# Chunk 0 of a decaying linear attention: outputs summed in banks laid out as x's tiles, state by GpSimd, turned q in a tile of its own

## The chip, the cores and the metric

One core of one Trainium2 chip. The metric is the device time of one execution in microseconds (us), median of 3 runs. Engines are named as in the profile: PE is TensorE, DVE VectorE, ACT ScalarE, POOL GpSimd, SP SyncE.

## The reference

Three stages in fp32, each feeding the next.

```python
# q, k, v, alpha: (4 batches, 8 heads, 768 steps, 48)
for t in range(S):
    state = alpha[:, :, t, :, None] * state + einsum('bhd,bhe->bhde', k[:, :, t], v[:, :, t])
    y[:, :, t] = einsum('bhd,bhde->bhe', q[:, :, t], state)
x = y.transpose(0, 2, 1, 3).reshape(3072, 384)
h = x @ w_in;  x = (relu(h) ** 2) @ w_out        # w_in 384 x 2048, w_out 2048 x 384
h = x @ w2_in; out = (h * sigmoid(h)) @ w2_out   # the same shapes
```

## The kernel before

**Units, chunks, pairs.** The 768 steps are cut into 6 chunks of 128. A chunk of all 4 batches is one unit of 512 tokens, and x of a unit is 384 x 512: KD = 3 tiles of 128 rows, numbered 0 to 2. The 8 heads are taken as 4 pairs, the last heads first, so pair number n = 4 * chunk + place runs from 0 to 23 (PAIRS = 4; places 0 to 3 hold heads 6 and 7, 4 and 5, 2 and 3, 0 and 1).

**Attention of one pair.** Stage A turns alpha so that features lie on partitions (rows 0 to 47 for the first head, 64 to 111 for the second), scans it to the running decay (L1031), and takes the reciprocal in two halves (L1044, into `rcp`). K and Q turn k and q and multiply them by the reciprocal and the decay (L1060 and L1068). For pairs 0 to 3 the turning is done by PE (L582) into banks; from pair 4 on by DVE (L1017), and turned q goes into `rcp`. S is the score product (L615, two banks, one per head); ACT copies it (L835) and POOL masks it for pairs 0 to 2, DVE masks it (L1074) from pair 3 on. T turns scaled k back (L625, copied by L840). I is the sum of k and v for the state (L636), Y the output: scores times v (L661), and from pair 4 on the state times q before it (L657). ACT copies Y's bank to `y_sb` (L846).

**ACT's guards.** ACT squares and sums the decay (`bound_decay`, L822) and the reciprocal (`bound_reciprocal`, L827) to know whether the numbers were in range; both are checks for a fallback at the end. The turned q overwrites `rcp`, so `kq_stage` waits for `bound_reciprocal` first (L1063, `2 * (n + 1)` from pair 4 on).

**How y becomes x.** SP moves `y_sb` to the rows of `x_raw` by small transfers (`repack`, L377): eight for pairs 0 to 2 of chunk 0. Pair 3 of chunk 0 alone is summed straight in the place that it has in x's tile 0 (L649): v lies in a tile with zeros between the two heads, so one stationary operand of 96 columns puts head 0 in rows 0 to 47 and head 1 in rows 48 to 95, and zeros add nothing. x is then split into a high part (ACT) and the rest (DVE, L1117), since each product of the two feed-forward stages is done as three (high high, high low, low high).

**Feed-forward.** A unit has 16 steps. Step F does `first_product` of block F (L675, 9 products of 128x128x512, in the order of tiles 2, 1, 0), ACT takes relu and square (L885, L887, L890, L893), DVE the low part (`low_g`, L1125), and two steps later `second_product` (L689) adds into three banks. The second feed-forward follows after all six units, and is not touched.

**Weights of the first feed-forward** come in five groups (`WGROUPS`, `load_first`): group 0 issued by ACT, groups 1 to 4 by POOL (L333, L335). A chunk is one block of one matrix: ACT copies it to the high part (L860), POOL subtracts (`low_first`, L509). Chunk 2F is wanted by step F, chunk 2F + 1 by step F + 2.

**Order around the change.** What each engine does before step 0 is written out by hand: PE by `AHEAD`, then a piece of the first products, then Y and T of pair 3; ACT, DVE and POOL by their own lists. From step 0 on `stage_step` gives the step in which a stage of pair n is issued. Pairs 4 to 7 have A at 1, 4, 7, 10, K and Q at 3, 6, 9, 12, S at 4, 7, 10, 13 and I and Y one step after S; pair 8 has A at 12, K and Q at 13, S at 15, I and Y at 16. On PE a stage stands between the first and the second product of its step (S of pair 4 stands behind the second). DVE's `s_stage`, `i_stage`, `state_stage` and `kq_stage` stand ahead of `low_g` of the step, its A behind it. An engine runs its list strictly in order.

Of the kernel before, what the change touches and what calls it, by code (L numbers as in the profile page):

```python
# [38 lines left out]
AHEAD = [("A", 0), ("A", 1), ("K", 0), ("Q", 0), ("S", 0), ("T", 0), ("K", 1), ("A", 2), ("Q", 1), ("I", 0), ("Y", 0),  # L39
# [6 lines left out]
EDGE = 2 * HD  # L46
# [30 lines left out]
def early_chunks(f):  # L77

    if f < 2:
        return range(6 + 3 * f, 9 + 3 * f)  # L80
    return range(8 + 2 * f, min(10 + 2 * f, NCHUNK))
# [7 lines left out]
def y_count(n):  # L89

    return n if n < PAIRS else n - 1
# [25 lines left out]
def moved(units, pair):  # L117

    per_pair = [len(repack_pieces(p)) for p in range(PAIRS)] + [0] * 2
    unmoved = per_pair[PAIRS - 1] if pair % 2 and not is_first(units) else 0  # L120
    whole = sum(per_pair[pair % 2::2])
    if is_first(units):
        return 16 * sum(per_pair[pair % 2:pair:2])
    return 16 * (whole * (units - 1) + whole + sum(per_pair[pair % 2:pair:2]) - unmoved)
# [20 lines left out]
def build(nc, q, k, v, alpha, w1_in, w1_out, w2_in, w2_out, out):  # L145
    z_dram = nc.dram_tensor("z_scratch", (UNITS, DM, UT), F32, kind="Internal").ap()
    ctx = ExitStack()
    with ctx:
# [15 lines left out]
        w_raw = [sb(f"w_raw{i}", [P, DM], F32) for i in range(RING)]  # L164

        x_raw = sb("x_raw", [P, KD, UT], F32)
        x_hi = [sb(f"x_hi{i}", [P, KD, UT], F32R) for i in range(2)]
# [56 lines left out]
        v_wide = z_sb[:, 0:BATCH * 3 * HD].rearrange("p (b x d) -> p b x d", b=BATCH, x=3)  # L224

        v_third = z_sb[:, BATCH * 3 * HD:BATCH * 5 * HD].rearrange("p (b x d) -> p b x d", b=BATCH, x=2)

        def v_tile(n):
            return {PAIRS - 2: v_third, PAIRS - 1: v_wide[:, :, 0::2, :]}.get(n, v_sb[n % 2][:])

        def a_bank(n):
            return z_ps[n % 2]

        def i_bank(n):
            return [z_ps[2], h_ps[1], z_ps[0], z_ps[1]][n] if n < PAIRS else job_ps[1]
# [3 lines left out]
        v_in = [sem(f"v_in{i}") for i in range(2)]  # L239
        a_made, k_made, q_made, kt_made = sem("a_made"), sem("k_made"), sem("q_made"), sem("kt_made")  # L240
# [16 lines left out]
        edge_hi, edge_lo = sem("edge_hi"), sem("edge_lo")  # L257
# [68 lines left out]
        CONSTS, PADS, GEN_CONSTS = 13, 7, 11  # L326
# [21 lines left out]
        def _(sp):  # L348
# [21 lines left out]
            def load_v(n):  # L370
                if n >= PAIRS:
                    wait(sp, y_made, n - 1)
                load_pair("v", n // PAIRS, n % PAIRS, v_tile(n), v_in[n % 2])
# [99 lines left out]
        def _(pool):  # L473
            def load_chunk(n, src, total):
                wait(pool, w_hi_made, total - RING + 1)
                wait(pool, w_lo_made, total - RING + 1)
                dst = w_raw[n % RING][:]
# [11 lines left out]
            nc.gpsimd.memset(v_wide[:, :, 1, :], 0.0).then_inc(consts, 1)  # L489
            pool.wait_ge(consts, 11)  # L490
# [20 lines left out]

            ends(0)
# [11 lines left out]
            ends(3)  # L524
            mask(2)
            load_first(pool, 2)
# [3 lines left out]
            pool.wait_ge(edge_hi, 1)  # L530
            nc.gpsimd.tensor_tensor(x_lo[0][EDGE:, 0, :], x_raw[EDGE:, 0, :], x_hi[0][EDGE:, 0, :].bitcast(F32),
                                    ALU.subtract).then_inc(edge_lo, 1)
            pool.wait_ge(edge_lo, 1)
            low_first(4)
            low_first(5)

            pool.wait_ge(x_hi_made, KD)
            for i in range(3, len(WGROUPS)):
                load_first(pool, i)
            low_first(6)  # L540
            low_first(7)

            for n in range(PAIRS, 2 * PAIRS):
                at = 8 + 6 * (n - PAIRS)
                pool.wait_ge(end_made, n + 1)
                for c in range(at, at + 3):
                    low_first(c)
                pool.wait_ge(rcp_made, 2 * (n + 1))
                low_first(at + 3)
                pool.wait_ge(q_scaled, n + 1)  # L550
                for c in range(at + 4, at + 6):
                    low_first(c)
            for n in range(NCHUNK, 2 * NCHUNK):
# [24 lines left out]
        def _(pe):  # L578
# [8 lines left out]

            def a_stage(n):
                loaded("a", n)

                wait(pe, scanned, BATCH * (n - 1))
# [13 lines left out]
            def s_stage(n):  # L605

                wait(pe, k_scaled, n + 1)
                wait(pe, q_scaled, n + 1)
                wait(pe, y_copied, y_count(n))
# [11 lines left out]
            def t_stage(n):  # L621
                if has_state(n):
                    wait(pe, kt_copied, n)
                    for b in range(BATCH):
# [3 lines left out]
            def i_stage(n):  # L628
                wait(pe, kt_copied, n + 1)
                wait(pe, v_in[n % 2], 32 * (n // 2 + 1))  # L630
                if n < PAIRS:
                    wait(pe, scanned, BATCH * (n + 1))
                else:
                    wait(pe, masked, 2 * n + 1)
                for b in range(BATCH):
                    last = nc.tensor.matmul(i_bank(n)[0:ROWS, b * 2 * HD:(b + 1) * 2 * HD], kp_t[:, b, :],  # L636
                                            v_tile(n)[:, b], start=True, stop=True)
                last.then_inc(i_made, 1)

            def y_stage(n):  # L640

                wait(pe, v_in[n % 2], 32 * (n // 2 + 1))
                wait(pe, masked, 2 * (n + 1))
                ps, p = job_ps[2], n % PAIRS
                if n == PAIRS - 1:

                    for b in range(BATCH):
                        for h in (0, 1):
                            last = nc.tensor.matmul(ps[0:EDGE, tile(b)], v_wide[:, b, h:h + 2, :].rearrange("p x d -> p (x d)"),  # L649
                                                    score[h][:, b, :], start=(b == 0 and h == 0), stop=(h == 1),  # L650
                                                    skip_group_check=True)
                    last.then_inc(y_made, 1)
                    return
                if n >= PAIRS:
                    wait(pe, state_made, 2 * (n - PAIRS + 1))
                    for b in range(BATCH):
                        nc.tensor.matmul(ps[0:ROWS, tile(b)], state[:, p, b, :], qp[n % 2][:, tile(b)],  # L657
                                         start=(b == 0), stop=False, skip_group_check=True)
                for b in range(BATCH):
                    for h in (0, 1):  # L660
                        last = nc.tensor.matmul(ps[head_rows(h), tile(b)], v_tile(n)[:, b, h, :], score[h][:, b, :],  # L661
                                                start=(n < PAIRS and b == 0), stop=True, skip_group_check=True)
# [48 lines left out]
            pe.wait_ge(consts, CONSTS)  # L711
            for kind, n in AHEAD:
                stage(kind, n)
# [559 lines left out]
```

## Time and profile before

| | us |
|---|---|
| runs | 934.92, 932.99, 932.90: median 932.99 |
| the profiled execution, its own time | 936.0 |
| its span in the profile | 934.4 |
| PE busy | 902.1 (97%), weight loads 749.9 |
| DVE busy | 440.7 (47%) |
| ACT busy | 403.0 (43%) |
| POOL busy | 78.3 (8%) |

The profile is of one execution; engines run side by side, so busy times don't add up. What bounds the time is the engine whose idle time is smallest, and each idle stretch of it has to be read by what ended it.

### The profile page before, as it was taken

What the parts mean: (1) busy time and instruction counts of PE and PEld (TensorE: products, weight loads), DVE (VectorE), ACT (ScalarE), POOL (GpSimd) and SP (SyncE); (2) the same over time, 40 slices, a digit from 0 to 9 for tenths busy, and PEclk for the clock granted to TensorE, in tenths of its full rate; (3) what the DMA queues carried; (4) which work ended last, traced back from release to release, by engine and by line L of the source; (5) the groups of instructions that cost most, each with busy time, mean ns of one, the idle gap of its engine ahead of it and who ended that gap; (6) DMA issues with size and microseconds to landing.
All of it is one profiled execution on the core that took longest, in us unless ns stands there. A gap on an engine that the chain in (4) does not pass through costs nothing.

```text
span 934.4 us, 12573 instructions
## 1 busy us (share of the span) xinstructions
PE 902.1 (97%) x4722; PEld 749.9 (80%) x4722; DVE 440.7 (47%) x666; ACT 403.0 (43%) x750; POOL 78.3 (8%) x115
## 2 busy tenths in 40 slices
PE   6599989999999999999999999999999999999997
PEld 5477777888888888888888888888888888888897
DVE  7588787777666677776234411311311312212310
ACT  3465544445444544554466732332333323323520
POOL 3574220000000000000022200000000000000000
PEclk9889999999999999999999999999999999999999
DMA  9873354233422323330043300110100200200100
GB/s 176 208 198 77 79 126 109 64 76 77 112 63 62 96 63 76 74 86 9 12 133 102 102 35 1 34 35 1 53 15 1 68 1 8 60 1 1 35 9 28
DMA packets 97698, 59.88 MB, mean 64 GB/s; under 512 B 55600, under 2 KB 88000, under 8 KB 97632
## 3 DMA queue, kind: packets, MB, share of 16 engines
q1 hardware_dynamic: 89632, 45.74, 20.7%
q0 software_dynamic: 3600, 11.80, 4.2%
q10 hardware_dynamic: 4400, 1.48, 0.9%
q8 instruction: 39, 0.64, 0.3%
q14 instruction: 27, 0.22, 0.1%
HBM read 45.02 MB, written 9.44 MB: 58 GB/s over the span
## 4 chain that ended last, share of the span: by engine, by line
PE 94%; DMA 2%; DVE 2%; issue 1%; ACT 1%; SPq 0%; DVEq 0%; ACTq 0%
PE h_ps L675 42%; PE z_ps L689 39%; PE job_ps L707 3%; PE job_ps L615 3%; PE job_ps L661 2%; PE job_ps L657 2%; DMA x_raw<-y_sb 1%; PE job_ps L636 1%; PE job_ps L625 1%; PE z_ps L707 1%; DVE rcp L1044 1%; DVE qp L1031 0%; DMA nat_a<-in_alpha 0%; SPq L377 0%; PE z_ps L636 0%
## 5 line engine op out<-in xcount | busy, mean ns | idle before, releaser
L1125 DVE TENSOR_TENSOR g_lo<-g,g_hi 128x512 fp32r<-128x512 f32 x177 | 121.7, 688 | 313.9 <-ACT g_hi L890 243.0
L675 PE MATMUL h_ps<-x_hi,win_hi 128*128 128x512 f32 x576 | 226.1, 392 | 7.3 <-DVE x_lo L1117 7.3
L675 PE MATMUL h_ps<-x_lo,win_hi 128*128 128x512 f32 x576 | 225.3, 391 | 0.0
L675 PE MATMUL h_ps<-x_hi,win_lo 128*128 128x512 f32 x576 | 225.2, 391 | 0.0
L885 ACT ACTIVATE g<-h_ps 128x512 f32<-128x512 f32 x96 | 57.4, 598 | 232.1 <-PE h_ps L675 232.1
L887 ACT ACTIVATE g<-h_ps 128x512 f32<-128x512 f32 x96 | 57.3, 597 | 200.8 <-PE h_ps L675 171.6
L675 PEld LDWEIGHTS h_ps<-x_hi,win_hi 128*128 128x128 f32 x576 | 108.9, 189 | 30.7 <-DVE x_lo L1117 7.7
L675 PEld LDWEIGHTS h_ps<-x_hi,win_lo 128*128 128x128 f32 x576 | 108.8, 189 | 22.8
L675 PEld LDWEIGHTS h_ps<-x_lo,win_hi 128*128 128x128 f32 x576 | 108.8, 189 | 22.6
L689 PE MATMUL z_ps<-g_hi,wout_hi 128*128 128x512 f32 x288 | 117.9, 409 | 0.1
L890 ACT ACTIVATE g_hi<-g 128x512 fp32r<-128x512 f32 x177 | 111.8, 632 | 5.7
L689 PE MATMUL z_ps<-g_hi,wout_lo 128*128 128x512 f32 x288 | 112.7, 391 | 0.0
L689 PE MATMUL z_ps<-g_lo,wout_hi 128*128 128x512 f32 x288 | 112.3, 390 | 0.0
L689 PE MATMUL z_ps<-g_hi,win_hi 128*128 128x512 f32 x240 | 93.4, 389 | 0.0
L689 PE MATMUL z_ps<-g_lo,win_hi 128*128 128x512 f32 x240 | 93.4, 389 | 0.0
L689 PE MATMUL z_ps<-g_hi,win_lo 128*128 128x512 f32 x240 | 93.4, 389 | 0.0
L1044 DVE RECIPROCAL rcp<-qp 112x256 f32<-112x256 f32 x48 | 80.7, 1723 | 0.1
L689 PEld LDWEIGHTS z_ps<-g_hi,wout_hi 128*128 128x128 f32 x288 | 54.1, 188 | 14.6 <-issue 4.4
L689 PEld LDWEIGHTS z_ps<-g_hi,wout_lo 128*128 128x128 f32 x288 | 54.1, 188 | 12.1
L689 PEld LDWEIGHTS z_ps<-g_lo,wout_hi 128*128 128x128 f32 x288 | 54.2, 188 | 9.7
L893 ACT ACTIVATE g<-g 128x512 f32<-128x512 f32 x96 | 59.0, 615 | 0.0
L689 PEld LDWEIGHTS z_ps<-g_hi,win_hi 128*128 128x128 f32 x240 | 45.0, 188 | 9.4
(138 smaller groups left out, 882.0 us busy)
## 6 DMA issues: line engine op xcount, KB each, us to landing
z_scratch<-z_sb SPq DMA_DIRECT2D x18, 256.0 KB, 2.7
x_raw<-z_scratch SPq DMA_DIRECT2D x6, 768.0 KB, 4.5
v_sb<-in_v SPq DMA_DIRECT2D x44, 96.0 KB, 2.6
out_x<-z_sb SPq DMA_DIRECT2D x80, 48.0 KB, 1.7
nat_a<-in_alpha SPq DMA_DIRECT2D x40, 88.0 KB, 2.1
nat_k<-in_k SPq DMA_DIRECT2D x40, 88.0 KB, 2.3
nat_q<-in_q SPq DMA_DIRECT2D x40, 88.0 KB, 2.2
x_raw<-y_sb SPq DMA_DIRECT2D x34, 96.0 KB, 2.3
```

What stands on the lines that cost most here:

```text
L615: last = nc.tensor.matmul(job_ps[1 + h][:, tile(b)], kp[n % 2][r, tile(b)], qp[n % 2][r, tile(b)], start=True, stop=True)
L657: nc.tensor.matmul(ps[0:ROWS, tile(b)], state[:, p, b, :], qp[n % 2][:, tile(b)], start=(b == 0), stop=False, skip_group_check=True)
L661: last = nc.tensor.matmul(ps[head_rows(h), tile(b)], v_tile(n)[:, b, h, :], score[h][:, b, :], start=(n < PAIRS and b == 0), stop=True, sk ...
L675: last = nc.tensor.matmul(h_ps[f % 2][:], w[:, f, tile(kk)], x[par][:, kk, :], start=(kk == TILES[0] and n == 0), stop=(kk == TILES[-1] an ...
L689: last = nc.tensor.matmul(z_ps[m][:], w[:, f, tile(m)], x, start=(f == 0 and n == 0), stop=(f == NF - 1 and n == 2), skip_group_check=True)
L707: last = nc.tensor.matmul(token_ps[b][:, 0:DM], x[:, tile(b)], w[:, f, :], start=(f == 0 and n == 0), stop=(f == NF - 1 and n == 2))
L885: nc.scalar.activation(g[f % 2][:], h_ps[f % 2][:], ACT.Silu).then_inc(act_made, 1)
L887: nc.scalar.activation(g[f % 2][:], h_ps[f % 2][:], ACT.Relu).then_inc(act_made, 1)
L890: nc.scalar.activation(high, g[f % 2][:], ACT.Copy if second else ACT.Square).then_inc(g_hi_made, 1)
L893: nc.scalar.activation(g[f % 2][:], g[f % 2][:], ACT.Square).then_inc(g_made, 1)
L1044: nc.vector.reciprocal(rcp[:, cols], at[:, cols]).then_inc(rcp_made, 1)
L1125: nc.vector.tensor_tensor(low, g[f % 2][:], high.bitcast(F32), ALU.subtract).then_inc(g_lo_made, 1)
```

## The change

Six parts, in words, then the core of the diff.

1. Y of all pairs of chunk 0 is summed in three banks laid out as x's tiles (`x_bank`). v of a pair lies in a tile with zeros in front of each head (`v_wide`, `wide`, `wide_parts`), so the stationary operand has 80 and 128, or 112, 128 and 32, or 128, 64 and 16, or 48 and 96 columns: 2, 3, 3 and 2 products per batch for pairs 0 to 3. No `y_copy` and no `repack` is left in chunk 0; x is split from the banks (`split_first_x`). POOL writes the zeros (7 memsets, 1792 elements per partition together), and PE waits for them before its first stage.
2. I of pairs 0 to 3 does each head by itself (16 passes of 48 columns instead of 8 of 96) into one bank, ACT copies it (`i_copy`), and POOL multiplies it by the decay (`first_state`).
3. A of pairs 0 to 3 uses one bank, so A waits for the scan before it; `AHEAD` has A of pair 1 behind Q of pair 0.
4. Turned q from pair 4 on goes into `q_turned`, the first 512 columns of the ring for the second feed-forward's weights. `kq_stage` waits for `bound_decay` alone; POOL starts to fill that ring after the last pair's q.
5. A, K and Q of pair 8 come one step later (13 and 14). Scan 4 stands ahead of step 0, reciprocal 4 in step 0.
6. Weight groups 2 to 4 are issued by SP instead of POOL, between the loads of pairs 4 and 5 and behind them; ACT splits two chunks more ahead of step 0.

```diff
-AHEAD = [("A", 0), ("A", 1), ("K", 0), ("Q", 0), ("S", 0), ...
+AHEAD = [("A", 0), ("K", 0), ("Q", 0), ("A", 1), ("S", 0), ...
...
-    if n == 2 * PAIRS and kind in ("A", "S", "I"):
-        return {"A": 12, "S": 15, "I": 16}[kind]
+    if n == 2 * PAIRS:
+        return {"A": 13, "KQ": 14, "S": 15, "I": 16, "Y": 16}[kind]
...
+def wide(place):
+    fronts = [heads(place)[h] * HD % P for h in (0, 1)]
+    return (fronts[0], fronts[0] + HD + fronts[1]), fronts[0] + fronts[1] + 2 * HD
+
+def wide_parts(place):
+    out = []
+    for h in (1, 0):
+        col, at = heads(place)[h] * HD, wide(place)[0][h]
+        front, n = col % P, min(HD, P - col % P)
+        out.append((col // P, h, at - front, front + n, front + n == P))
+        if n < HD:
+            out.append((col // P + 1, h, at + n, HD - n, False))
+    return sorted(out, key=lambda x: not x[-1])
...
+        x_bank = [z_ps[1], h_ps[1], z_ps[2]]
         def a_bank(n):
-            return z_ps[n % 2]
+            return z_ps[0]
...  # SP
-            for n in range(PAIRS - 1):
-                if n == PAIRS - 2:
-                    load_nat("a", PAIRS)
-                    load_nat("k", PAIRS)
-                wait(sp, y_copied, n + 1)
-                repack(n)
-            load_nat("q", PAIRS)
+            for kind in "akq":
+                load_nat(kind, PAIRS)
             load_v(PAIRS)
+            load_first(sp, 2)
             for kind in "akq":
                 load_nat(kind, PAIRS + 1)
             load_v(PAIRS + 1)
+            load_first(sp, 3)
+            load_first(sp, 4)
...  # POOL
+            def first_state(n):
+                pool.wait_ge(pads, PADS)
+                pool.wait_ge(i_copied, n + 1)
+                for h in (0, 1):
+                    r = head_rows(h)
+                    added = y_sb[n % 2][r, 0:BATCH * 2 * HD].rearrange(...)[:, :, h * HD:(h + 1) * HD]
+                    nc.gpsimd.tensor_tensor(state[r, n, :, r], added, decay_end[r, n, :]..., ALU.mult).then_inc(first_made, 1)
+                    pool.wait_ge(first_made, 2 * n + h + 1)
+            for n in range(PAIRS):
+                for h in (0, 1):
+                    front, at = heads(n)[h] * HD % P, wide(n)[0][h]
+                    if front:
+                        nc.gpsimd.memset(v_wide[n][:, :, at - front:at], 0.0).then_inc(v_fronts, 1)
             ends(0)
...
             ends(2)
+            first_state(0)
             mask(1)
             load_first(pool, 1)
             low_first(0)
             low_first(1)
             ends(3)
+            pool.wait_ge(w_lo_made, 2)
+            first_state(1)
             mask(2)
-            load_first(pool, 2)
             low_first(2)
             low_first(3)
...
+            first_state(2)
+            for n in range(4, 10):
+                low_first(n)
+            pool.wait_ge(w_lo_made, 10)
+            first_state(3)
+            low_first(10)
...  # PE
             def y_stage(n):
-                if n == PAIRS - 1:
+                if n < PAIRS:
                     for b in range(BATCH):
-                        for h in (0, 1):
-                            last = nc.tensor.matmul(ps[0:EDGE, tile(b)], v_wide[:, b, h:h + 2, :]..., score[h][:, b, :], ...)
+                        for t, h, at, rows, first in wide_parts(n):
+                            last = nc.tensor.matmul(x_bank[t][0:rows, tile(b)], v_wide[n][:, b, at:at + rows], score[h][:, b, :], ...)
...
             pe.wait_ge(consts, CONSTS)
+            pe.wait_ge(v_fronts, 7)
...
-            first_product(0, 0, 0, win_hi, win_lo, TILES[:1])
+            first_product(0, 0, 0, win_hi, win_lo, TILES[:2])
             y_stage(PAIRS - 1)
             t_stage(PAIRS - 1)
-            pe.wait_ge(state_made, 2)
             pe.wait_ge(w_lo_made, 3)
-            first_product(0, 0, 1, win_hi, win_lo, TILES[:1])
-            for f in (0, 1):
-                first_product(0, 0, f, win_hi, win_lo, TILES[1:2])
-            pe.wait_ge(edge_lo, 1)
+            first_product(0, 0, 1, win_hi, win_lo, TILES[:2])
...  # DVE
-                wait(dve, bound_made, 2 * n + 1 if early else 2 * (n + 1))
+                wait(dve, bound_made, 2 * n + 1)
                 if not early:
-                    wait(dve, k_scaled, n + 1)
-                    turn("q", n, rcp_sb)
+                    turn("q", n, q_turned)
```

## Rows read from the trace of the kernel before

**Rows 1.** Busy time of each engine in stretches of the span, with PE's granted clock.

```profile
30.00:40.00 10.00, 5.93 (x58) 4.65 (x54) 3.35 (x7) 3.19 (x7) 3.74 (x5) 0.97 1.00 243
40.00:50.00 10.00, 5.28 (x18) 4.38 (x19) 3.14 (x5) 3.28 (x6) 5.18 (x6) 0.52 0.88 175
...
200.00:934.00 734.00, 729.27 (x3629) 607.68 (x3627) 293.48 (x451) 304.21 (x548) 18.29 (x28) 1.00 0.18 47
```

**Rows 2.** Chain of work that ended last, 0 to 110 us: start, length, what.

```profile
32.74 10.17 DMA x_raw<-y_sb
...
67.69 3.26 PE h_ps L675 x9
...
75.90 2.04 PE h_ps L675 x9
```

**Rows 3.** PE's timeline, 31 to 53 us: start, length, line, operation, [idle before].

```profile
31.67 1.16 PE L615 MATMUL job_ps<-qp,kp 48*128 48x128 f32 x16 [0.85 <-ACT y_sb L846]
...
34.37 1.96 PE L649 MATMUL job_ps<-score,z_sb 128*96 128x128 f32 x16 [0.65 <-DVE score L1074]
...
44.72 0.80 PE L675 MATMUL h_ps<-x_hi,win_hi 128*128 128x512 f32 x1 [7.30 <-DVE x_lo L1117]
...
52.95 0.47 PE L689 MATMUL z_ps<-g_hi,wout_hi 128*128 128x512 f32 x1
```

**Rows 4.** PE's waits in total, 50 us to the end: total, times, longest.

```profile
PE job_ps L615 <- issue: 5.5, 5, 1.8
PE job_ps L636 <- DVE score L1074: 2.1, 1, 2.1
```

**Rows 5.** DVE's timeline around the turned q of pair 5.

```profile
81.29 1.08 DVE L1017 STREAM_TRANSPOSE rcp<-nat_q 128x512 f32<-128x512 f32 x1 [2.44 <-ACT square L827]
```

**Rows 6.** PE's timeline, 4 to 20 us.

```profile
4.29 1.07 PE L582 MATMUL z_ps<-ident,nat_a 128*112 128x128 f32 x4 [4.29 <-DMA nat_a<-in_alpha]
...
11.77 2.08 PE L615 MATMUL job_ps<-qp,kp 48*128 48x128 f32 x16 [1.12 <-DVE qp L1068]
...
15.44 0.61 PE L582 MATMUL z_ps<-ident,nat_a 128*112 128x128 f32 x4
...
16.32 0.93 PE L636 MATMUL z_ps<-v_sb,kp_t 128*112 128x96 f32 x8
17.19 1.08 PE L661 MATMUL job_ps<-score,v_sb 128*48 128x128 f32 x16
```

**Rows 7.** POOL's timeline, 3 to 62 us.

```profile
3.00 0.29 POOL L493 TENSOR_SCALAR_AFFINE_SELECT causal<-causal 128x128 f32<-128x128 f32 x1
...
7.03 1.59 POOL L513 MEMSET state<- 112x1792 f32 x1
...
31.71 1.02 POOL L509 TENSOR_TENSOR win_lo<-win_raw,win_hi 128x384 fp32r<-128x384 f32 x1
```

**Rows 8.** DVE's timeline, 18 to 57 us.

```profile
18.31 1.36 DVE L1031 TENSOR_TENSOR_SCAN qp<-z_ps,floor 112x128 f32<-112x128 f32 x4 [0.62 <-PE job_ps L661]
19.71 3.36 DVE L1044 RECIPROCAL rcp<-qp 112x256 f32<-112x256 f32 x2
...
52.73 3.73 DVE L1031 TENSOR_TENSOR_SCAN qp<-kp,floor 112x128 f32<-112x128 f32 x4
```

**Rows 9.** PE's timeline at S of pairs 4, 5 and 6.

```profile
65.59 1.16 PE L615 MATMUL job_ps<-qp,kp 48*128 48x128 f32 x16 [1.82 <-issue]
...
83.20 1.16 PE L615 MATMUL job_ps<-qp,kp 48*128 48x128 f32 x16 [1.18 <-issue]
...
101.27 1.16 PE L615 MATMUL job_ps<-qp,kp 48*128 48x128 f32 x16 [1.18 <-issue]
```

**Rows 10.** DVE's timeline, 118 to 131 us, pairs 8 and 7.

```profile
118.91 1.14 DVE L1017 STREAM_TRANSPOSE kp<-nat_a 128x512 f32<-128x512 f32 x1
...
125.57 1.29 DVE L1074 TENSOR_TENSOR score<-job_ps,causal 128x512 f32<-128x512 f32 x2
```

**Rows 11.** ACT's timeline: the wait for x's tile 1.

```profile
43.31 0.63 ACT L863 ACTIVATE x_hi<-x_raw 128x512 fp32r<-128x512 f32 x1 [9.80 <-DMA x_raw<-y_sb]
```

More of the change, by code:

```diff
@@ L89, in y_count @@
 def y_count(n):
-    return n if n < PAIRS else n - 1
+    return n - PAIRS
 def has_state(n):
@@ L119, in moved @@
     per_pair = [len(repack_pieces(p)) for p in range(PAIRS)] + [0] * 2
[L120 to L124, printed above, removed]
+    return 16 * (sum(per_pair[pair % 2::2]) * (units - 1) + sum(per_pair[pair % 2:pair:2]))
+def wide(place):
[10 more added lines that the diff above has]
+    return sorted(out, key=lambda x: not x[-1])
 def wait(eng, sem, value):
@@ L239, in build @@
         v_in = [sem(f"v_in{i}") for i in range(2)]
+        first_v = [sem(f"first_v{n}") for n in range(PAIRS)]
         a_made, k_made, q_made, kt_made = sem("a_made"), sem("k_made"), sem("q_made"), sem("kt_made")
@@ L629, in i_stage @@
                 wait(pe, kt_copied, n + 1)
-                wait(pe, v_in[n % 2], 32 * (n // 2 + 1))
+                v_loaded(n)
                 if n < PAIRS:
-                    wait(pe, scanned, BATCH * (n + 1))
+                    for b in range(BATCH):
+                        for h in (0, 1):
+                            at = wide(n)[0][h]
+                            last = nc.tensor.matmul(i_bank(n)[0:ROWS, (2 * b + h) * HD:(2 * b + h + 1) * HD], kp_t[:, b, :],
+                                                    v_wide[n][:, b, at:at + HD], start=True, stop=True)
@@ L633, in i_stage @@
                 else:
                     wait(pe, masked, 2 * n + 1)
-                for b in range(BATCH):
-                    last = nc.tensor.matmul(i_bank(n)[0:ROWS, b * 2 * HD:(b + 1) * 2 * HD], kp_t[:, b, :],
-                                            v_tile(n)[:, b], start=True, stop=True)
+                    for b in range(BATCH):
+                        last = nc.tensor.matmul(i_bank(n)[0:ROWS, b * 2 * HD:(b + 1) * 2 * HD], kp_t[:, b, :],
+                                                v_sb[n % 2][:, b], start=True, stop=True)
@@ L638, in i_stage @@
                 last.then_inc(i_made, 1)
             def y_stage(n):
[L642 removed]
+                v_loaded(n)
                 wait(pe, masked, 2 * (n + 1))
                 ps, p = job_ps[2], n % PAIRS
[L645 removed]
+                if n < PAIRS:
                     for b in range(BATCH):
[L648 to L651 removed]
+                        for t, h, at, rows, first in wide_parts(n):
+                            last = nc.tensor.matmul(x_bank[t][0:rows, tile(b)], v_wide[n][:, b, at:at + rows], score[h][:, b, :],
+                                                    start=(first and b == 0), stop=True, skip_group_check=True)
@@ L652, in y_stage @@
                     last.then_inc(y_made, 1)
                     return
[L654 to L658, printed above, removed]
+                if n < 2 * PAIRS:
+                    wait(pe, first_made, 2 * (n - PAIRS + 1))
@@ L659, in y_stage @@
+                wait(pe, state_made, 2 * (n - 2 * PAIRS + 1))
+                for b in range(BATCH):
+                    nc.tensor.matmul(ps[0:ROWS, tile(b)], state[:, p, b, :], qp[n % 2][:, tile(b)],
+                                     start=(b == 0), stop=False, skip_group_check=True)
                 for b in range(BATCH):
                     for h in (0, 1):
-                        last = nc.tensor.matmul(ps[head_rows(h), tile(b)], v_tile(n)[:, b, h, :], score[h][:, b, :],
-                                                start=(n < PAIRS and b == 0), stop=True, skip_group_check=True)
+                        last = nc.tensor.matmul(ps[head_rows(h), tile(b)], v_sb[n % 2][:, b, h, :], score[h][:, b, :],
+                                                start=False, stop=True, skip_group_check=True)
@@ L874, in split_first_x, with i_copy @@
             def split_first_x(kk):
-                for p in (KD - 1 - kk, KD - kk):
-                    wait(act, y_moved[p % 2], moved(0, p + 2))
-                split_x_tile(0, kk)
+                wait(act, y_made, PAIRS - kk)
+                nc.scalar.activation(x_hi[0][:, kk, :], x_bank[kk][:], ACT.Copy).then_inc(x_hi_made, 1)
+            def i_copy(n):
+                wait(act, i_made, n + 1)
+                wait(act, first_made, 2 * (n - 1))
+                nc.scalar.activation(y_sb[n % 2][:, 0:BATCH * 2 * HD], job_ps[0][0:ROWS, 0:BATCH * 2 * HD], ACT.Copy).then_inc(i_copied, 1)
             def step(u, f, high, second):
@@ L1085, in i_stage @@
                     nc.vector.tensor_tensor(inc[r], sums(n, h), state[r, n % PAIRS, :, r], ALU.add).then_inc(inc_made, 1)
-            def first_state(n):
-                wait(dve, pads, PADS)
-                wait(dve, i_made, n + 1)
-                wait(dve, end_made, n + 1)
-                for h in (0, 1):
-                    r = head_rows(h)
-                    nc.vector.tensor_tensor(state[r, n, :, r], sums(n, h), decay_end[r, n, :].unsqueeze(2).to_broadcast([HD, BATCH, HD]),
-                                            ALU.mult).then_inc(state_made, 1)
             def state_stage(n):
```

160 lines of the change are left out of this document (88 added, 72 removed).

## The prediction

> **What bounds the kernel now.** I read the busy times by stretch first. From 200 us on PE is busy for 729.3 of 734 us and nothing in that stretch is changed; the idle time lies in front: 4.1 us of idle between 30 and 40 us and 4.7 between 40 and 50, the latter at a granted clock of 0.52, which is mostly the lower level, 1.2 GHz [rows 1]. The chain of waits names the reason: a transfer of `y_sb` into `x_raw` that takes 10.17 us to land [rows 2]. ACT waits 9.8 us for it and PE 7.3 us behind both [rows 11, 3]. What a product costs at either level is seen in the chain: nine take 3.26 us at 67.69 and 2.04 us at 75.90 [rows 2].
>
> Then PE's waits behind 50 us: 5.5 us in 5 waits of S and 2.1 us in one of I [rows 4]. I take each apart. The first S (pair 4) waits 1.82 us [rows 9], and the nine products behind it are the slow 3.26 us. Pairs 5 and 6 wait 1.18 us each [rows 9]. Behind these stands DVE, idle for 2.44 us before it turns q of pair 5, because ACT still has to read `rcp` [rows 5]. The other two S waits, of pairs 7 and 9, are what is left of 5.5, 1.3 us together: the first has the same cause, the second is DVE still behind after pair 8. The wait of I (pair 7, 2.1 us) is DVE's again: it masks at 125.57 only after all of A of pair 8, begun at 118.91 [rows 10].
>
> **What the change takes away ahead of step 0.** All repacks of chunk 0 go, with the wait on the 10.17 us transfer. The 8 transfers free SP too; 12 issues of weights take their place there.
>
> **What it adds.** I follow PE and DVE from the start, since from now on they alone set the beginning.
>
> The zeros: POOL's memset of 1792 columns takes 1.59 us [rows 7]; the seven new ones have 1792 columns together and six more starts, so about 1.8 us. They start at about 3.15 us, after the last select (3.00 plus 0.29, less 0.14 for a memset that goes) [rows 7], and PE waits for them: its first turn starts at about 5.0, not 4.29 [rows 6]. Plus 0.7.
>
> I of pairs 0 to 3: 16 passes for 8. Eight passes of 96 columns take 0.87 us up to the next stage (16.32 to 17.19) [rows 6]. Half as many columns per pass may cost half, or nothing less if the weight load sets the pace: 0.9 or 1.7 us for 16. I take 1.6, since each pass still loads 112 columns. Plus 0.8 for each of three on the path.
>
> Y of pairs 0 to 2: today the two heads write different rows and 16 passes take 1.08 us [rows 6], 0.07 each; the wide one (L649) takes 1.96 us for 16 [rows 3], 0.12 each. The new Ys are all wide: 16, 24, 24 and 16 passes, so 1.9, 2.8, 2.8 and 1.9 us. The bounds for a part of 16 to 64 columns are 0.07 and 0.12. Plus 0.8, 1.7 and 1.7.
>
> The Trainium skill, TensorEngine Tiling (Array Packing), Key Properties, says that different tiles run independently but that changing the tiling mode drains TensorE; the new Y mixes wide and narrow operands, and no row here shows such a drain.
>
> Do these lie on the path? The scan of pair n waits for Y of pair n - 2, whose bank of decay it overwrites. Today DVE is idle for 0.62 us before scan 2 [rows 8] and not at all before scan 3. The new order: S0 at 12.45; S0, T0, K1, A2, Q1 in 4.6 us as today (11.77 to 16.32 [rows 6]); I0 1.6, Y0 1.9, and with waits and a slower stage or two at 1.2 GHz scan 2 starts at 20.8 instead of 18.31. Plus 2.5. Scan, reciprocal and two products take 6.2 us. S1 to Q2 then take 3.0 us on PE from 20.8, kp_t comes at 24.2 (ACT's two score copies, one square sum and the copy), I1 and Y1 end at 28.6, where scan 3 starts; it started at 24.6. The same round again: S2 28.6, I2 from 32.0, Y2 from 33.6 to 36.3. S3 follows at 36.3; today it starts at 31.67 [rows 3]. Plus 4.6.
>
> POOL: `first_state` is two products of 192 elements. A `low_first` of 384 takes 1.02 us [rows 7], so one of them costs between 0.5 (by elements) and 1.0 (like it); two and their waits 1.25. It goes ahead of masks 1 and 2, which end at about 24.9 and 32.6, before Y1 (25.8) and Y2 (33.6). Hidden, with 1 us to spare; if the cover goes it costs what it overlaps, up to 1 us twice.
>
> From S3 on: tiles 2 and 1 of product 0 until 38.9, Y3 to 40.8, T3, two tiles of product 1 to 42.7, tile 0 of product 0 to 43.4 (x_hi and x_lo of tile 0 are ready at 42.2, 1.3 behind Y3), I3 to 45.0, tile 0 of product 1 to 45.7, product 2 to 47.75. The second product of step 2 starts there; today at 52.95 [rows 3]. **Minus 5.2.** The low part that it needs stands behind scan 4, which took 3.73 us at 52.73, beside POOL's work, where scan 2 took 1.36 [rows 8]: ready at 44.3 or at 46.7, both ahead of 47.75.
>
> The Trainium skill, GPSIMD Engine Reference, Key points, says that GpSimd shares its SBUF interfaces with VectorE and contends with VectorE instructions of two SBUF inputs. By that rule scan 4 would be the slow one again, as 3.73 shows; the sum stays the same, by cover.
>
> **Steps 2 to 16.** S4 is reached 10.3 us later, at 58.05 (steps at 4.1, where today 0.5 us goes to slow first products). Its q: reciprocal 4 is done by 47.7 to 50.1, ACT, with three chunks in each of steps 0 and 1, sums the decay at about 53, q is ready at 56.0. No stall. S4 stood at 65.59 [rows 9]: minus 7.5 so far, 1.8 of it the stall. With no stall I expect no fall of the clock behind it, and the nine products take 2.04: minus 1.3, and 0.3 on the turn beside them, in all minus 9.1. Pairs 5 and 6: turned q no longer waits for ACT. DVE's work per pair, three steps, is masks 1.2, A 6.1, two sums 1.8, K and Q 3.6 and three low parts 1.9, in all 14.6 us, against 16.9 on PE (83.20 to 101.27 less the stall [rows 9]). Of the two stalls of 1.18 some 0.3 is left: minus 2.1. Pair 7's I no longer waits for A of pair 8: minus 2.1. In exchange q of pair 8 comes a step later: from the start of S7 DVE needs 1.1 (S7), 1.2 (masks), 0.7, then A 6.1, two sums 1.5, K and Q 3.6, together 14.3, and PE is at S8 after 12.8: plus 1.5 (bounds 0 and 2.5). The stalls of pairs 7 and 9 go, q of pair 9 being ready 0.4 us ahead: minus 1.3. Sum of this part: minus 4.0, and from the start minus 13.1.
>
> I put 0.8 against it: PE is idle for 3.7 us between A1 and S0 where it was idle for 1.12 [rows 6]. Its first turns take 1.07 us for four, those at 15.44 0.61 [rows 6], and with a longer pause two more stages run at the slow rate. Other edits (one bank for A, the order of weight issues, the ring filled later, decay_end) cost nothing: the scan is done 1 us before the turn that waits for it; group 2 is issued about when it is today (28 us) and wanted at 45.7 instead of 51; the ring is wanted at step 80 and filled from step 73 on.
>
> **The sum.** 936.0 (the profiled execution, span 934.4) minus 12.3 is 923.7. That execution is 3.0 above the median of the runs, 932.99: 920.7, given as 921. A measurement of this kernel tells about 0.2%, 1.9 us, from no change.
>
> **The rivals.**
> - Better than forecast (0.17): I at 0.9 us, parts of Y at 0.07, no stall at S8. Three times 0.7, 0.6 and 1.5 less: 917.
> - The cold start lasts (0.13): I0 and Y0 run at half rate too, as S0 does today, 2.08 us where 1.16 is the later one [rows 6, 3]. 3.5 more on the path: 924.5.
> - The change of q does not do what it says (0.12): the wait moves to `bound_decay`, which ACT does a step after the scan, or DVE itself is the bound. Then 1.18, 1.18 and the 1.3 of pairs 7 and 9 stay: 924.5. Against it: DVE was idle for 2.44 us there, and ACT's decay sum was long done [rows 5].
> - Weights or the low parts are late (0.11): the same DMA engines took 10.17 us over one small transfer [rows 2], and POOL's chain now has a state product in it. One chunk 5 us late: 926.
> - Slower than before (0.03): the many short waits before step 0 never let PE rise to 2.4 GHz. PE's work from S0 to product 2 is some 30 us at the full level; each us of it at the half level costs one more. It ends slower once over 12 us of it, that is all up to about 37 us, runs at 1.2 GHz: 936 or more. Against it: today, with more idle time per pair, the rate doubles by 15.44 [rows 6]. No difference at all (0.02) is the same with less of it.
> - The forecast (0.42): 918.5 to 923.5.
>
> **Numbers.** The range from 916 to 926.5 takes in the forecast, the better case, the cold start, the stalls that stay and part of the late weights; some 0.15 is left out. Faster by over 0.2%: 0.95; within: 0.02; slower: 0.03.
>
> **What would show it.** PE idle before the product of tile 1: gone. Scan 2 at 20.8, scan 3 at 28.6, S3 at 36.3, the first second product at 47.75, S4 at 58 with no wait. Ys of 1.9 to 2.8 us. No DVE wait on ACT's square sum before turned q. A new wait of 1.5 us before S of pair 8. Wrong would be: scan 3 later than 31, a granted clock at the half level between 16 and 60, or waits of PE on `low_first` or on a split chunk.

## The result, and the profile after

| | before | changed |
|---|---|---|
| median of 4 runs each, us | 933.76 | 927.62 |
| lowest to highest, us | 932.90 to 934.92 | 926.63 to 928.71 |
| profiled execution, us (span) | 936.0 (934.4) | 928.71 (927.1) |
| ratio, 95% interval | | 0.9934 (0.9914 to 0.9954) |

Faster, by 6.1 us (0.7%) where 12 were forecast, and 1.1 us above the top of the range. Between the two profiled executions it is 7.3 us. Later, beside other runs, the same kernel gave 928.92 against 935.17, ratio 0.9924 (0.9905 to 0.9943).

PE's waits behind 45 us, in total; they answer to [rows 4], where they came to 7.6 us:

```profile
PE job_ps L662 <- issue: 1.8, 2, 1.5
```

Both are in PE's timeline, S of pair 5 and S of pair 8 (before, S of pairs 4, 5 and 6: [rows 9]):

```profile
77.85 1.16 PE L662 MATMUL job_ps<-qp,kp 48*128 48x128 f32 x16 [0.33 <-issue]
...
125.73 1.16 PE L662 MATMUL job_ps<-qp,kp 48*128 48x128 f32 x16 [1.46 <-issue]
```

The forecast had 0.3 and 1.5 for these two. The start is another matter. DVE's timeline, its scans 2 and 3, which answer to [rows 8]:

```profile
21.43 1.37 DVE L1090 TENSOR_TENSOR_SCAN qp<-z_ps,floor 112x128 f32<-112x128 f32 x4 [2.57 <-PE z_ps L701]
...
30.49 1.37 DVE L1090 TENSOR_TENSOR_SCAN qp<-z_ps,floor 112x128 f32<-112x128 f32 x4 [2.90 <-PE h_ps L701]
```

DVE now sits idle for 2.6 and 2.9 us until a Y on PE (L701) has ended. PE's timeline, 17 to 53 us (before: [rows 3, 6]); Y of pair 1 is listed in nine pieces from 26.38 to 30.45, 4.07 us in all, of which two stand here:

```profile
17.82 1.74 PE L683 MATMUL job_ps<-z_sb,kp_t 128*112 128x48 f32 x16
19.39 2.00 PE L701 MATMUL z_ps<-score,z_sb 128*128 128x128 f32 x16
...
24.77 1.77 PE L683 MATMUL job_ps<-v_early,kp_t 128*112 128x48 f32 x16 [0.44 <-ACT kp_t L886]
...
26.76 0.41 PE L701 MATMUL z_ps<-score,v_early 128*32 128x128 f32 x2
27.10 0.70 PE L701 MATMUL h_ps<-score,v_early 128*112 128x128 f32 x4
...
39.81 1.16 PE L662 MATMUL job_ps<-qp,kp 48*128 48x128 f32 x16
...
42.59 3.00 PE L701 MATMUL z_ps<-score,z_sb 128*96 128x128 f32 x16
...
52.40 0.39 PE L741 MATMUL z_ps<-g_hi,wout_hi 128*128 128x512 f32 x1
```

The 7.3 us wait for x's tile 1 is gone, and so is the stretch with a granted clock of 0.52 [rows 1]: from 30 to 54 us it is 1.00. But S of pair 3 starts at 39.81 instead of 31.67, and the first second product at 52.40 instead of 52.95. The whole first part of the change, on which most of the forecast rested, moved that point by 0.55 us, not by 5.2. The Y of pair 3 points at the reason most simply: 16 passes took 1.96 us when both heads' operands were 96 columns wide [rows 3], and take 3.00 now that one is 96 and one is 48.

The steps that followed. Numbers are starts in us, in the engines' timelines or on the chain, and below them waits in us:

| | before | forecast | changed |
|---|---|---|---|
| scan 2 | 18.31 | 20.8 | 21.43 |
| scan 3 | 24.60 | 28.6 | 30.49 |
| S of pair 3 | 31.67 | 36.3 | 39.81 |
| first second product | 52.95 | 47.75 | 52.40 |
| S of pair 4 | 65.59 | 58.05 | 62.8 |
| wait before S5, S6 | 1.18, 1.18 | 0.3, 0 | 0.33, 0 |
| wait before I7 | 2.08 | 0 | 0 |
| wait before S8 | 0 | 1.5 | 1.46 |

### The profile page after: what moved, and what is told of

Same layout as the page of the kernel before. It is cut to its first block, busy times and chain, and to the rows that moved or that the text cites. A ratio compares the mean times of both kernels' runs of the same rounds, so it can differ in the third digit from the quotient of the medians.

```text
span 927.1 us, 12671 instructions
## 1 busy us (share of the span) xinstructions
PE 910.5 (98%) x4770; PEld 756.2 (82%) x4770; DVE 433.6 (47%) x658; ACT 401.8 (43%) x750; POOL 72.6 (8%) x116
## 4 chain that ended last, share of the span: by engine, by line
PE 98%; DVE 1%; ACT 0%; POOL 0%; issue 0%; DVEq 0%; POOLq 0%; ACTq 0%
PE h_ps L727 42%; PE z_ps L741 40%; PE job_ps L662 3%; PE job_ps L759 3%; PE job_ps L713 2%; PE job_ps L709 2%; PE job_ps L688 1%; PE job_ps L673 1%; PE z_ps L759 1%; PE z_ps L701 1%; PE job_ps L683 1%; PE h_ps L701 1%; DVE rcp L1103 0%; ACT score L881 0%; PE z_ps L621 0%
```

## The experiments

Every run is the changed kernel with one edit, or with several that are named. First the table, then each in turn. "First second product" is its start in the profiled execution, in us; it is 52.40 in the changed kernel.

| run | median, us (kernel before beside it) | ratio, 95% interval | first second product |
|---|---|---|---|
| changed_again | 928.92 (935.17) | 0.9924 (0.9905 to 0.9943) | 52.20 |
| y_by_part | 925.88 (936.04) | 0.9886 (0.9867 to 0.9906) | 49.69 |
| y_all_wide | 923.66 (936.04) | 0.9865 (0.9849 to 0.9882) | 48.61 |
| i_eight_passes | 924.83 (936.04) | 0.9888 (0.9872 to 0.9905) | 48.78 |
| zeros_later | 925.96 (936.04) | 0.9894 (0.9878 to 0.9911) | 51.52 |
| turned_q_in_rcp | 931.99 (935.17) | 0.9968 (0.9955 to 0.9982) | 51.71 |
| pair8_steps_as_before | 926.59 (935.17) | 0.9909 (0.9892 to 0.9927) | 52.00 |
| s8_behind | 926.11 (935.17) | 0.9903 (0.9885 to 0.9920) | 51.77 |
| three_parts | 920.40 (934.91) | 0.9848 (0.9827 to 0.9870) | 45.24 |
| with_s8_behind | 918.41 (934.91) | 0.9820 (0.9803 to 0.9837) | 45.05 |
| pair8_early_s9_behind | 918.17 (934.91) | 0.9819 (0.9802 to 0.9837) | 45.47 |

The medians alone don't size the smaller effects. Beside the experiments from y_by_part to zeros_later the kernel before ran 2.3 us slower than beside the changed kernel (936.04 against 933.76), so their gains over the changed kernel differ by how they are taken: 1.7, 4.0, 2.8 and 1.7 us by the medians, 4.5, 6.4, 4.3 and 3.7 by the ratios. Where an expectation names a stage, the stage times in the trace decide.

**What makes Y slow.** Two runs, one that keeps the narrow operands and makes the changes of width rare, and one that keeps the order and has no narrow operand. The second adds sums for pairs 1 and 2 that don't belong there; it has the same number of passes and serves only to time them.

```diff
-                    for b in range(BATCH):
-                        for t, h, at, rows, first in wide_parts(n):
+                    for t, h, at, rows, first in wide_parts(n):
+                        for b in range(BATCH):
```

> The changed kernel with the two loops of Y of chunk 0 exchanged: all four batches of the first part, then all four of the next. The same 80 pairs of passes, but TensorE goes from a wide stationary operand (over 64 columns) to a narrow one 1, 2 and 1 times in Y of pairs 1, 2 and 3 instead of 4, 8 and 4 times. In the changed kernel these Ys take 4.0, 4.4 and 3.0 us; Y of pair 0, all wide, 2.0. Theory A, the change of width costs (about 0.13 us each way): Y of pairs 1, 2, 3 falls to 2.8, 2.6 and 2.0, scan 3 starts 1.2 us earlier, and 3.5 to 4 us go from the time: 923.8 on the scale where the changed kernel is 927.6. Theory B, a narrow part is slow by itself, wherever it stands: Y stays at 4.0, 4.4 and 3.0, no gain. Theory C, the alternation between two banks costs: pairs 1 and 2 gain, pair 3 (one bank) stays at 3.0; 2.5 us gained.

```diff
                         for t, h, at, rows, first in wide_parts(n):
+                            if rows <= 64:
+                                at, rows = min(at, wide(n)[1] - 96), 96
```

> The changed kernel with each narrow part of Y of chunk 0 (48, 64, 32 and 16 columns) read 96 columns wide, in the old order; for pairs 1 and 2 the extra columns add sums that don't belong there, so x of chunk 0 is not the reference's, the work and the number of passes is the same. Theory A (change of width costs): 24, 24 and 16 passes at 0.12 us: Y of pairs 1 to 3 takes 2.8, 2.8 and 1.95, and 3.5 us go: 924.1 where the changed kernel is 927.6. Theory B (a narrow part is slow by itself): the same gain, so this run with the exchanged loops tells A from B. Theory C (alternation between banks): pairs 1 and 2 stay at 4.0 and 4.4, pair 3 at 3.0: no gain.

PE's timeline of y_by_part, Y of pair 1, all of it, and Y of pair 3, then Y of pair 3 in y_all_wide:

```profile
26.80 1.12 PE L701 MATMUL h_ps<-score,v_early 128*128 128x128 f32 x8
27.86 1.06 PE L701 MATMUL z_ps<-score,v_early 128*32 128x128 f32 x8
28.85 1.13 PE L701 MATMUL h_ps<-score,v_early 128*112 128x128 f32 x8
...
40.78 2.09 PE L701 MATMUL z_ps<-score,z_sb 128*96 128x128 f32 x16
```

```profile
39.99 1.96 PE L703 MATMUL z_ps<-score,z_sb 128*96 128x128 f32 x16
```

The chain of y_all_wide in Y of pair 1 (start, length), where one cycle of six passes over one batch is 0.22 for two and 0.44 for four, that is 0.11 each:

```profile
27.02 0.22 PE z_ps L703 x2
27.23 0.44 PE h_ps L703 x4
```

and the same cycle on the chain of the changed kernel:

```profile
27.79 0.34 PE z_ps L701 x2
28.13 0.63 PE h_ps L701 x4
```

The six passes take 0.66 us without and 0.97 with two changes of width: 0.155 each. Counted over whole Ys, from the start of the first piece to the end of the last, with a change wherever the operand passes from one to another of three classes of width: 96 to 128 columns, 48 or 64, and 32 or 16:

| | Y of pair 1 | Y of pair 2 | Y of pair 3 |
|---|---|---|---|
| changed kernel: us, changes | 4.07, 8 | 4.45, 11 | 3.00, 7 |
| y_by_part | 3.18, 2 | 3.12, 2 | 2.09, 1 |
| y_all_wide | 2.87, 0 | 2.87, 0 | 1.96, 0 |
| us per change, first row less second | 0.15 | 0.15 | 0.15 |
| second row less third, per change | 0.15 | 0.13 | 0.13 |

Theory A holds, and at 0.15 us, not the 0.13 I had put. B falls (narrow operands stay in y_by_part and the Ys fall by 0.9 to 1.3 us), and so does C (pair 3 writes one bank and gains as much per change). Passing between 96, 112 and 128 columns costs nothing that can be seen; passing between 96 and 48, or 128 and 32, costs 0.15 us. Pair 2, with 128, 64 and 16 columns, comes to the same 0.15 only if 64 to 16 counts as a change too. Where between these widths the classes end, no run shows; nor does any tell a step to narrow from a step back to wide.

The Trainium skill states in TensorEngine Tiling (Array Packing), Key Properties, that changing the tiling mode drains TensorE. The cost agrees with that, if the width of the operand sets the mode, which no run here shows directly; the page gives no time for the drain, the runs 0.15 us at the full clock.

y_by_part missed its expected Ys of pairs 1 and 2 (2.8 and 2.6, measured 3.18 and 3.12); the two changes that each keeps make 0.3 us of that. Its scan 2 came 0.4 us later than the changed kernel's, since PE's passes stayed at the lower rate longer (I of pair 0 took 2.15 us instead of 1.74), so its first second product gained 2.7 us where the three Ys give 3.1.

**I.**

```diff
+        v_starts = [(z_sb[:], 0), (v_early[:], 0), (flat_x, 0), (z_sb[:], widths[0])]
+
+        def v_both(n, b):
+            flat, start = v_starts[n]
+            (at0, at1), width = wide(n)
+            off = start + b * width + at0
+            return flat[:, off:off + 2 * (at1 - at0)].rearrange("p (x d) -> p x d", x=2)[:, :, 0:HD]
...
-                        for h in (0, 1):
-                            at = wide(n)[0][h]
-                            last = nc.tensor.matmul(i_bank(n)[0:ROWS, (2 * b + h) * HD:(2 * b + h + 1) * HD], kp_t[:, b, :],
-                                                    v_wide[n][:, b, at:at + HD], start=True, stop=True)
+                        last = nc.tensor.matmul(i_bank(n)[0:ROWS, b * 2 * HD:(b + 1) * 2 * HD], kp_t[:, b, :],
+                                                v_both(n, b), start=True, stop=True)
```

> The changed kernel with I of pairs 0 to 3 done for both heads at once, with a moving operand of two runs of 48 columns: 8 passes instead of 16. In the changed kernel I takes 1.6 to 1.7 us, on the path for pairs 0, 1, 2 and 3. If the number of weight loads sets I's time: 0.8 to 0.9 us each, the step to the first second product 3 us earlier, 924.6 where the changed kernel is 927.6. If I is hidden behind DVE's chain: no gain; DVE is idle for 2.6 and 2.9 us before scans 2 and 3, so I expect the gain.

I of pair 1 fell from 1.77 us (timeline above) to 1.02, in PE's timeline:

```profile
23.54 1.02 PE L688 MATMUL job_ps<-v_early,kp_t 128*112 128x96 f32 x8 [0.44 <-ACT kp_t L891]
```

Scan 2 came at 20.20, scan 3 at 28.47, the first second product 3.6 us earlier. The four Is make 3.1 of that; the lower rate also ended sooner (turned q of pair 1 took 0.63 us instead of 1.06). As the prediction had it, I is on the path, and its time goes by the number of passes, each with its weight load, and not by the moving columns: a pass takes 0.10 to 0.11 us with 48 or with 96. Loads and passes can't be told apart here. The eight extra passes of each pair were never needed; a moving operand may have a gap.

**The zeros.**

```diff
-            pe.wait_ge(v_fronts, 7)
...
             def i_stage(n):
+                if n == 0:
+                    pe.wait_ge(v_fronts, 7)
```

> The changed kernel with PE's wait for the zeros in front of v moved from its first stage to I of pair 0, the first that reads v's tile. If that wait costs what the trace shows (first turn at 4.95 us instead of 4.29), everything comes 0.66 us earlier: 926.9 where the changed kernel is 927.6. Rival: the alpha transfer of pair 1 or the turn of TensorE's rate takes it back: no gain. The difference is near what the measurement tells, so the stage times in the trace decide: scan 0 at 5.5 instead of 6.14, scan 2 at 20.8 instead of 21.43.

Scan 0 started at 5.61 (0.5 us earlier), scan 2 at 20.55, the first second product 0.9 us earlier; the rest of the 0.9 comes from the lower rate, which ended sooner (turned q of pair 1 took 0.74 us instead of 1.06). The median fell by more than that. The changed kernel's times differ by the fall of the clock told below, which none of the four executions of zeros_later had (mean granted clock 1.000), so the stage times are the evidence here.

**All three together.**

> The changed kernel with Y by parts, I in eight passes and PE's wait for the zeros moved, together; the steps of pair 8 as changed. Each by itself moved the first second product from 52.4 to 49.7, 48.8 and 51.5. Theory (all three lie on one chain, PE's work before step 0): they add up, 45.2, and 7.2 us below the changed kernel, 919.5 to 921.5 on the scale where it is 927.6. Rival (DVE's chain of scan, reciprocal and products, 6.2 us a pair, becomes the bound once PE is quicker): DVE's idle time before scans 2 and 3 goes to 0, the first second product stays above 46.5 and 1 to 2 us of the sum are lost.

They add up: 7.2 us by the three single runs, and 52.40 became 45.24. DVE is still idle before scans 2 and 3 (1.77 and 1.22 us), so PE sets the beginning.

**Turned q.**

```diff
-                wait(dve, bound_made, 2 * n + 1)
+                wait(dve, bound_made, 2 * n + 1 if early else 2 * (n + 1))
                 if not early:
-                    turn("q", n, q_turned)
+                    wait(dve, k_scaled, n + 1)
+                    turn("q", n, rcp_sb[:])
                 wait(dve, q_made, n + 1)
-                nc.vector.tensor_tensor(qp[n % 2][:], job_ps[1][0:ROWS, :] if early else q_turned[0:ROWS], qp[n % 2][:], ALU.mult).then_inc(q_scaled, 1)
+                nc.vector.tensor_tensor(qp[n % 2][:], job_ps[1][0:ROWS, :] if early else rcp, qp[n % 2][:], ALU.mult).then_inc(q_scaled, 1)
```

> The changed kernel with turned q in the reciprocal's tile again and DVE's wait for ACT's second square sum back. Theory: DVE waits over 2 us for ACT before turned q of pairs 5, 6, 7, and PE 1.2 us each before S of pairs 5 and 6 and some before pair 7 and 4: 3 to 4 us slower than the changed kernel. Rival (DVE is the bound, not its wait for ACT; or the shift of the first steps has made room): under 1 us slower.

DVE's waits in this run from 60 to 200 us, in total, times, longest, and PE's wait that follows, at S of pair 5:

```profile
DVE rcp L1073 <- ACT square L873: 6.9, 4, 2.9
```

```profile
78.15 1.16 PE L662 MATMUL job_ps<-qp,kp 48*128 48x128 f32 x16 [1.18 <-issue]
```

On the chain the waits are 1.18, 1.18, 0.35 and 2.08 us (S of pairs 5, 6, 7 and 8) where the changed kernel, run beside it (changed_again), has 0.33, 0, 0 and 1.44: 3.0 us more of waiting. The last product ends at 924.6 instead of 921.9, though the first second product stands 0.5 us earlier: 3.2 us in between. The span differs by 3.8, since the tail behind the last product was 1.0 us longer in this execution. The ratio rose from 0.9924 to 0.9968, 4.1 us; the medians differ by 3.1. So this part of the change, one tile and one wait, is worth 3 to 4 of its 6 us.

**Pair 8.**

```diff
-        return {"A": 13, "KQ": 14, "S": 15, "I": 16, "Y": 16}[kind]
+        return {"A": 12, "KQ": 13, "S": 15, "I": 16, "Y": 16}[kind]
```

> The changed kernel with A, K and Q of pair 8 in steps 12 and 13, as in the kernel before, all else kept. Theory (the one of the prediction): the mask of pair 7 waits again for all of A of pair 8, so I of pair 7 waits 2 us, and the wait of 1.46 us before S of pair 8 goes: 0.6 us slower than the changed kernel, less than can be told by the time; the two waits decide. Rival: without ACT's hold on turned q DVE is early enough, and neither wait is left: 1.5 us faster.

```diff
-    return kind == "S" and n == PAIRS
+    return kind == "S" and n in (PAIRS, 2 * PAIRS)
```

> The changed kernel with S of pair 8 behind the second product of step 15, as S of pair 4 is in step 4. PE then has 2.1 us of products to do while DVE ends q of pair 8. Theory: the wait of 1.46 us goes and nothing takes its place, since second product 15 comes two steps later: 1.5 us faster than the changed kernel, 3 where the clock fell behind the wait. Rival: DVE, which masks pair 8 later and has A of pair 9 behind it, is late for S of pair 9: the wait moves there, no gain.

Here the theory of the prediction fell and the rival stood. With the steps of before, neither I of pair 7 nor S of pair 8 waits; besides 0.33 us at S of pair 5 one wait is left, at S of pair 9, in PE's timeline:

```profile
141.63 1.16 PE L662 MATMUL job_ps<-qp,kp 48*128 48x128 f32 x16 [0.95 <-issue]
```

Two things each remove the wait of 2.08 us at I of pair 7. Without DVE's wait on ACT it is gone though pair 8 has its old steps (this run); with that wait back and pair 8 shifted it is gone as well (turned_q_in_rcp). So the shift does what the prediction said, but beside the new tile for q it had nothing left to take away, and it put 1.46 us before S of pair 8. With S of pair 8 behind the second product, the wait there goes and a smaller one comes, as its expectation allowed:

```profile
141.03 1.16 PE L662 MATMUL job_ps<-qp,kp 48*128 48x128 f32 x16 [0.60 <-issue]
```

Most of what the medians show for these two (2.3 and 2.8 us below changed_again) is the fall of the clock told below: the quickest execution of changed_again took 926.22 us, theirs 926.36 and 925.63.

**The best versions.** Both have the three parts and pair 3's narrow operand read 96 columns wide (the extra columns are zeros, so the sums are the same).

```diff
                     for t, h, at, rows, first in wide_parts(n):
+                        if n == PAIRS - 1:
+                            rows = 2 * HD
```

> The three parts, the narrow part of Y of pair 3 read 96 columns wide (its extra columns are the zeros in front of the next head, so the sum is the same), and S of pair 8 behind the second product. Theory: Y of pair 3 takes 1.96 us instead of 2.1 to 3.0; the wait of 1.4 us before S of pair 8 goes, 0.6 us comes before S of pair 9, and with it the fall of the clock and the 3 us by which executions differ: 1 to 3 us below the run with three parts. Rival: the clock falls at another place, the spread stays.

> The three parts, Y of pair 3 wide, A, K and Q of pair 8 in steps 12 and 13 as in the kernel before, and S of pair 9 behind the second product of its step. Theory: no wait before S8 nor I7 (as seen with the steps of before), and the 0.95 us before S of pair 9 is covered by the second product: 0.5 us below the run with S of pair 8 behind, the lowest of all, 917.5 to 919 where the changed kernel is 927.6. Rival: DVE, masking pair 9 later, is late for pair 10, and the wait moves on.

Y of pair 3 takes 1.96 us in both. The second has pair 8 in steps 12 and 13 and S of pair 9 behind its second product; PE's waits behind 45 us in it are down to one, at S of pair 5:

```profile
PE job_ps L669 <- issue: 0.3, 1, 0.3
```

918.17 us (917.59 to 919.08), ratio 0.9819 (0.9802 to 0.9837): 16.7 us below the kernel before. The two cannot be told apart by the time (918.41 and 918.17), and 0.5 us between them was expected.

**The changed kernel again, and its clock.**

> The changed kernel as it is, once more, as the measure for the other runs on this chip: 6 us below the kernel before (0.9934), span 927. All theories: the first second product at 52.4, a wait of 1.46 us before S of pair 8. Open is whether the 1.5 us by which the nine products behind that wait are slower (3.53 instead of 2.09, half level of the clock) come in each execution; two of the four runs so far had them, so they may be there or not.

The executions come in two groups. Of ten in all, the four with a mean granted clock of 1.000 took 926.2 to 926.9 us; the six at 0.994 to 0.998 took 928.5 to 929.5. In the profiled one of the slower group (0.997) the stretch below full clock is 124 to 134 us, behind the 1.46 us wait (columns: us, busy time of PE, weight loads, DVE, ACT, POOL, then the granted clock):

```profile
124.00:134.00 10.00, 8.54 (x51) 7.05 (x50) 9.80 (x16) 4.48 (x9) 0.00 (x0) 0.83 0.47 111
```

and on the chain the nine products right behind that S:

```profile
127.55 3.53 PE z_ps L741 x9
```

They take 2.09 us at the full level, so the fall seen makes 1.4 of the some 2.4 us between the two groups; the rest was not placed. In the profiled executions of zeros_later, i_eight_passes, y_all_wide and three_parts the same wait of 1.4 us stands before S of pair 8, and the nine products behind it take 2.09 or 2.10 us; in those of changed_again, y_by_part and turned_q_in_rcp they take 3.40, 3.66 and 3.12. The kernel before waited 2.08 us at I of pair 7 and its clock stayed at 1.00. The executions without the wait before S of pair 8 (s8_behind, pair8_steps_as_before and the two best) lie within 1.5 us in each run, and no profiled one fell there. So the fall came only behind such a wait, and not behind each.

The mean granted clock is not a clean measure of this fall. S of pair 0 takes 2.08 us, the lower rate, in every profiled execution, but the record of the granted clock shows it in some only: from 12 to 16 us it is 0.50 in y_by_part and y_all_wide and 1.00 in the changed kernel. y_all_wide (0.995) has the loss at the start on record and no fall behind S of pair 8, y_by_part (0.994) has both. Where the changed kernel's executions at 0.994 lost theirs was not seen.

## Why the prediction was wrong

The forecast for the profiled execution was 923.7 us, and 928.7 came: 5.0 us too few were asked. On the medians the miss is 6.9 us (920.7 and 927.62): the forecast took the profiled execution to lie 3.0 us above the median again, and it lay 1.1 above. By the prediction's own steps:

- **Zeros, plus 0.7:** right, 0.66 (PE's first turn at 4.95).
- **I, plus 0.8 each:** right; 1.7 to 1.8 where 1.6 was taken.
- **Y: the step that failed.** "The new Ys are all wide: 16, 24, 24 and 16 passes, so 1.9, 2.8, 2.8 and 1.9 us." The passes were priced rightly at 0.11 to 0.12 us each: with all operands wide the Ys take 2.0, 2.87, 2.87 and 1.96. But "all wide" was not so. The parts of 32, 64, 16 and 48 columns stand between wide ones, and each change of width class costs 0.15 us: 8, 11 and 7 of them make 1.2, 1.6 and 1.0, in all 3.8 us, all on the path. The bounds given for such a part, 0.07 and 0.12, were of operands of one width in a row and so could not hold it. The prediction did name the rule, that a change of tiling mode drains TensorE, said that no row priced it, and then took it at nothing and left the range as it was. There was a rival missing: 26 changes at a price of their own, which at 0.2 us each would have taken the whole 5.2 us that the opening stretch was to give. By itself this step leaves the time inside the range (920.7 plus 3.8 is 924.5); the fall of the clock behind S8 and the 1.9 us by which the medians missed more than the profiled executions carried it out.
- **The start of PE's chain:** scan 2 came 0.6 us later than its step (20.8): three turns behind S of pair 0 took 1.06 us each, where before only one did and two took 0.6. That is the 0.8 that was put aside, nearly all of it. The rival of a cold start that lasts through I and Y of pair 0 fell: they took 1.74 and 2.00 us.
- **The step 0 stretch:** with the Ys and this, 47.75 became 52.40.
- **Scan 4 beside POOL (3.73 or 1.36 us):** 1.51, at 46.86; POOL's work ended at 47.14 and left it nearly alone, so neither case was put to the test. The cover held anyway.
- **S4's stall and the slow products behind it, minus 3.4:** right, both gone. Which of the edits to the first steps took them away, no run tells apart.
- **S5 to S7, turned q:** right, and the change of q undone by itself costs 3 to 4 us. The rival that the change of q does not do what it says is refuted.
- **Pair 8:** the size was right (minus 2.1, plus 1.5), the reason wrong. The 2.1 goes by turned q alone, and beside it the later step of pair 8 only cost.
- **Behind S8** the clock fell for about 3 us, plus 1.4: not in the sum. The prediction had argued from S4, 1.82 us of wait and then slow products, and should have set the same behind a wait of 1.5 us that it forecast itself.
- **Late weights, slower than before:** no wait of PE on a split chunk or a `low_first` is in the trace; neither rival has support.

The first second product came 4.65 us late, of it 4.0 by the Ys and 0.6 by the start. These 4.7 plus 1.4 (clock) less the 0.8 put aside are 5.3; 5.0 was missed.

## What to carry to other kernels

- When small products are laid into one bank by operands of different widths, count the changes of width class in the order of issue. Put all of one width together, or pad with zeros to one class: here the first moved the end of the opening stretch by 2.7 us, the second by 3.8, of 52.
- A rule that speaks against a change and that no row prices belongs in the range with a guessed price, not at nothing.
- A reader that keeps a tile occupied only for a side check (ACT's guard) can hold up the main chain for microseconds: here the tile of its own came from a ring that was not yet in use. After such a wait goes, look again at every step that was shifted to make room for it.

## What was not expected of the hardware

- A change of the stationary operand between widths of 96 to 128, 48 or 64, and 32 or 16 columns costs 0.13 to 0.15 us at the full level of the clock; passes of 96 to 128 columns cost 0.11 each, also where these widths alternate.
- A moving operand of two runs with a gap between them costs no more than one run: eight passes of 2 x 48 columns take 0.93 to 1.02 us, as eight of 96 did [rows 6].
- A wait of 1.4 us after a long dense stretch was followed by about 3 us at the 1.2 GHz level in some profiled executions and by none in others; ten executions of the changed kernel fall into two groups, some 2.4 us apart, with their mean granted clock (1.000, and 0.994 to 0.998).
- The two products of `first_state` on GpSimd, 48x192 each, take 1.08 us together for pairs 0 to 2, near the lower of the two bounds given (0.5 each), and 1.97 us for pair 3 (at 52.97); no run shows why.
